# Tile 0's attention reordered, and the halves of the first weight blocks given to other engines and slots

## The reference

```python
scores = scale * q @ k.T                    # 2 batches, 8 heads, 768 rows, head size 64
keep = (key < n_global) | ((0 <= row - key) & (row - key < n_local))   # 8 and 96
a = softmax(where(keep, scores - slope[h] * dist, -1e9))
x = (a @ v)                                 # laid out as 1536 x 512
h = x @ w_in                                # 512 -> 1024
s = h * softmax(h)
y = (s - mean(s)) / sqrt(var(s) + 1e-6) * g_ln @ w_out      # 1024 -> 512
yn = y / sqrt(mean(y * y) + 1e-6) * rms_g
out = (silu(yn @ w_gate) * (yn @ w_val)) @ w_down           # 512 -> 1536 -> 512
```

## Time and profile before

| what | value |
|---|---|
| median of 3 runs | 596.89 us (596.87 to 596.99) |
| profiled execution, its own time | 597.28 us |
| its span | 595.5 us |
| PE busy | 575.6 us (97%) |
| DVE, ACT, POOL busy | 303.3, 258.4, 83.5 us |
| mean granted clock of PE | 0.977 |

### The profile page before, as it was taken

How to read it: one execution, slowest core, us unless ns; L and a number is a source line. 1 busy time by engine, 2 the same in 40 slices (tenths; PEclk the granted TensorE clock), 3 DMA queues, 4 the chain that set the end, 5 groups by cost and what they waited for, 6 DMA issues and landing times.

```text
span 595.5 us, 10886 instructions
## 1 busy us (share of the span) xinstructions
PE 575.6 (97%) x3787; PEld 520.8 (87%) x3787; DVE 303.3 (51%) x778; ACT 258.4 (43%) x598; POOL 83.5 (14%) x223
## 2 busy tenths in 40 slices
PE   6967999999999999999999999999999999999997
PEld 6956888888888888878899999999999999999996
DVE  5757878777877898767455213222222222221211
ACT  3655656665665677646454212222221222222112
POOL 4440220222112205213010010001001000100000
PEclk9796799999999999999999999999999999999999
DMA  8664454432443343232532100020020000000000
GB/s 215 188 187 139 128 172 124 137 109 77 124 125 108 91 126 99 81 133 89 181 108 85 58 16 1 1 72 1 1 70 0 0 0 35 0 0 36 2 0 36
DMA packets 21614, 46.97 MB, mean 79 GB/s; under 512 B 2764, under 2 KB 2776, under 8 KB 21576
## 3 DMA queue, kind: packets, MB, share of 16 engines
q1 hardware_dynamic: 21264, 46.47, 25.9%
q10 hardware_dynamic: 312, 0.01, 0.0%
HBM read 40.18 MB, written 6.29 MB: 78 GB/s over the span
## 4 chain that ended last, share of the span: by engine, by line
PE 81%; DVE 9%; POOL 4%; issue 3%; ACT 2%; DMA 1%; ACTq 0%; DVEq 0%; SPq 0%
PE hidden L412 9%; PE hidden L413 9%; PE hidden L414 8%; PE mixed L1248 5%; PE turned L412 3%; PE turned L413 3%; PE mixed L412 3%; PE mixed L413 3%; PE scores_b L412 3%; PE scores_a L413 3%; PE scores_b L413 3%; PE scores_a L412 3%; PE turned L414 3%; PE scores_a L414 3%; PE scores_b L414 3%
## 5 line engine op out<-in xcount | busy, mean ns | idle before, releaser
L733 ACT ACTIVATE act_hi<-act_sb 128x256 fp32r<-128x256 f32 x72 | 30.2, 419 | 108.7 <-DVE act_sb L1106 108.7
L1106 DVE TENSOR_TENSOR act_sb<-mixed,silu 128x256 f32<-128x256 f32 x36 | 15.3, 425 | 93.3 <-PE mixed L414 93.1
L1106 DVE TENSOR_TENSOR act_sb<-turned,silu 128x256 f32<-128x256 f32 x36 | 15.3, 424 | 89.3 <-PE turned L414 86.8
L1248 PEld LDWEIGHTS mixed<-v_in,probs_t 116*128 116x128 f32 x384 | 53.4, 203 | 7.8 <-ACT probs_t L684 4.2
L684 ACT ACTIVATE probs_t<-turned 116x512 f32<-116x512 f32 x48 | 28.7, 598 | 67.6 <-PE turned L1233 67.5
L412 PE MATMUL hidden<-down_hi,act_hi 128*128 128x512 f32 x144 | 56.9, 395 | 0.1
L413 PE MATMUL hidden<-down_lo,act_hi 128*128 128x512 f32 x144 | 56.9, 395 | 0.0
L414 PE MATMUL hidden<-down_hi,act_lo 128*128 128x512 f32 x144 | 56.7, 393 | 0.0
L1248 PE MATMUL mixed<-v_in,probs_t 116*128 116x64 f32 x384 | 51.7, 281 | 3.4 <-ACT probs_t L684 3.4
L1111 DVE TENSOR_TENSOR act_lo<-act_sb,act_hi 128x256 fp32r<-128x256 f32 x72 | 30.6, 425 | 35.0 <-ACT act_hi L733 35.0
L674 ACT ACTIVATE probs<-logits,neg_max 128x232 f32<-128x232 f32 x96 | 45.8, 483 | 3.8 <-DVE neg_max L997 3.8
(11 more groups left out here) (147 smaller groups left out, 1567.5 us busy)
## 6 DMA issues: line engine op xcount, KB each, us to landing
qk_raw<-qk_pairs SPq DMA_DIRECT2D x96, 180.0 KB, 3.2
v_in<-v_windows SPq DMA_DIRECT2D x12, 448.0 KB
staging<-w_gate SPq DMA_DIRECT2D x3, 1024.0 KB, 7.3
staging<-w_val SPq DMA_DIRECT2D x3, 1024.0 KB, 5.8
y_spill<-y_out SPq DMA_DIRECT2D x12, 256.0 KB, 4.2
staging<-w_down SPq DMA_DIRECT2D x3, 1024.0 KB, 5.7
y_in<-y_spill SPq DMA_DIRECT2D x6, 512.0 KB, 4.0
out<-o_sb SPq DMA_DIRECT2D x12, 256.0 KB, 2.1
```

What stands on the lines that cost most here:

```text
L733: nc.scalar.activation(act_hi[:, slot], act_sb[:, slot], ACT.Copy).then_inc(act_rounded, 1)
L1106: nc.vector.tensor_tensor(act_sb[:, slot], val_ps[slot][:, 0:WIDE], silu[:, slot], ALU.mult).then_inc(act_ready, 1)
L1248: ins = pe.matmul(mixed[:, head * d:(head + 1) * d], probs_t[:, p % 2, h, half], v_in[:, even, half, head * d:(head + 1) * d], start=(half ...
```

## The change

- SP's queue begins with the DMA of n_local, which was ACT's second.
- `find_general` is the first thing that DVE computes after the bounds; ACT reads the flag before tile 0's first exp, not after it.
- In `one_tile(-1)` PE issues, for each pair, the scores of the next pair, 3 fillers, the transposes, 1 filler and the mix. Before it was transposes, scores, 3 fillers, mix, 3 fillers. In front of that, 6 fillers stand for 3.
- SP loads block 1 at the start of `one_tile(-1)` and not at its end.
- Blocks 0 and 1 are each split half by DVE and half by POOL. POOL does block 0's second half between the fourth and the fifth of the 8 biases, and block 1's second half behind them. DVE did both halves of block 0 before, POOL both of block 1.
- The four roundings of w_out, and so their splits on DVE, stand one pair later.
- `take_logits` of tile 1 waits for the two biases of its own pair and not for all eight.

```diff
@@ one_tile on PE
-                        turn_pair(n, p)
                         score_pair(n + 1, (p + 1) % pairs)
                         keep_busy(FILL)
+                        turn_pair(n, p)
+                        keep_busy(1)
                         mix_pair(a, 1 - even, p)
-                        keep_busy(FILL)
                         continue
@@ the start of PE
             score_pair(0, 0)
-            keep_busy(FILL)
+            keep_busy(2 * FILL)
@@ slots of roundings and splits
         round_1 = {(-1, 1): [(0, 0)], (-1, 2): [(0, 1)], (0, 0): [(1, 0), (1, 1)],
-                   (0, 2): [(2, 0)], (0, 3): [(2, 1)], (1, 0): [(3, 0)], (1, 1): [(3, 1)],
+                   (0, 3): [(2, 0)], (1, 0): [(2, 1)], (1, 1): [(3, 0)], (1, 2): [(3, 1)],
...
-        del split_1[0, 1]
+        del split_1[-1, 3]
+        split_1[0, 1] = [(1, 0)]
@@ POOL
+            def split_half(c):
+
+                hi, lo, raw, _ = half_block(c, 1)
+                pool.wait_ge(w_rounded, 2 * c + 2)
+                pool.tensor_tensor(lo, raw, hi.bitcast(F32), ALU.subtract).then_inc(w_in_split[c], 1)
...
-            for half in range(2):
-                hi, lo, raw, _ = half_block(1, half)
-                pool.wait_ge(w_rounded, 2 * 1 + half + 1)
-                pool.tensor_tensor(lo, raw, hi.bitcast(F32), ALU.subtract).then_inc(w_in1_split, 1)
+                if h == heads // 2 - 1:
+                    split_half(0)
+            split_half(1)
@@ SP
+            sp.dma_start(bounds_i[:, 1, :], n_local.bitcast(I32).partition_broadcast(P)).then_inc(bounds_in, 16)
...
+                if known(t) and t < 0:
+                    load_block(sp, 1)
                 for p in range(pairs):
...
-                if known(t) and t < 0:
-                    load_block(sp, 1)
@@ ACT
-            for i, n in enumerate((n_global, n_local)):
-                act.dma_start(bounds_i[:, i, :], n.bitcast(I32).partition_broadcast(P)).then_inc(bounds_in, 16)
+            act.dma_start(bounds_i[:, 0, :], n_global.bitcast(I32).partition_broadcast(P)).then_inc(bounds_in, 16)
...
-            exp_pair(0, 0, 0)
             act.wait_ge(general_known, 1)
             general = act.value_load(general_i[0:1, 0:1], min_val=0, max_val=1)
             with act.If(general != 0):
                 general_attention()
+            exp_pair(0, 0, 0)
@@ DVE
-                if known(n) and n == pairs:
-                    dve.wait_ge(bias_others, heads)
+                if known(n) and pairs <= n < 2 * pairs:
+                    dve.wait_ge(bias_others, 2 * (p + 1))
...
+            find_general()
             start_distance(0)
             split_qk(0, 0)
             finish_distance(0)
             set_bias()
             take_logits(0, 0, 0)
-            find_general()
             split_qk(1, 1)
```

More of the change, by code:

```diff
@@ L215, in fused_kernel @@
         w_split = sem("w_split")
-        w_in1_split = sem("w_in1_split")
+        w_in_split = [sem("w_in0_split"), sem("w_in1_split")]
         qk_loaded = [sem(f"qk_loaded_{p}") for p in range(pairs)]
@@ L337, in wait_split @@
         def wait_split(engine, c):
-            if c == 1:
-                engine.wait_ge(w_in1_split, 2)
+            if c < N1:
+                engine.wait_ge(w_in_split[c], 2)
             else:
-                engine.wait_ge(w_split, 2 if c == 0 else 2 * c)
+                engine.wait_ge(w_split, 2 * (c - N1 + 1))
         def load_block(sp, c):
@@ L387, in split_block @@
             if gain is None:
-                nc.vector.tensor_tensor(lo, raw, hi, ALU.subtract).then_inc(w_split, 1)
+                nc.vector.tensor_tensor(lo, raw, hi, ALU.subtract
+                                        ).then_inc(w_in_split[c] if c < N1 else w_split, 1)
                 return
@@ L846, in _, with find_general @@
                                            in1=bounds_f[:, :, 0], op0=ALU.mult, op1=ALU.add).then_inc(setup, 1)
+            def find_general():
+                dve.wait_ge(setup, 3)
+                nc.vector.tensor_scalar(general_f[:], bounds[:, 0:1], float(GLOBAL), None, ALU.is_gt).then_inc(setup, 1)
+                dve.wait_ge(setup, 4)
+                nc.vector.scalar_tensor_tensor(out=general_f[:], in0=bounds[:, 1:2], scalar=float(PREV + 1),
+                                               in1=general_f[:], op0=ALU.is_gt, op1=ALU.max).then_inc(setup, 1)
+                dve.wait_ge(setup, 5)
+                nc.vector.scalar_tensor_tensor(out=general_i[:], in0=bounds[:, 1:2], scalar=1.0,
+                                               in1=general_f[:], op0=ALU.is_lt, op1=ALU.max).then_inc(general_known, 1)
             DIST_STEPS = 7
-            DISTANCE = (3, 12)
             def start_distance(v):
-                at = DISTANCE[v]
+                at = 5 + DIST_STEPS * v
                 dve.wait_ge(iota_done, 7)
@@ L883, in set_bias @@
                                             ).then_inc(bias_first, 1)
[L885 to L893, removed]
             def general_attention():
```

## The result

The changed kernel took 603.33 us (median of 6, 599.68 to 605.16). Beside it the kernel before took 596.83 (median of 6); the ratio is 1.0107, with a 95% interval of 1.0069 to 1.0146. That is slower, as forecast, but by 6.4 us and not by 2.3, and outside the range. Timed beside the later variants the kernel before had medians of 595.3 to 596.2, lower than the three runs shown ahead of the prediction. So medians of different comparisons can't be subtracted to better than 1 or 2 us, and the ratios are the safe figures: 0.001 of ratio is 0.6 us.

The account below looks back on a forecast made before the run. PE was taken to bound the kernel from 80.57 us on, its milestones and clock deciding before; -0.6 + 1.8 - 3.4 - 2.5 + 0.5 + 3.3 + 3.2 = +2.3 gave 599.2 us, range 594.3 to 601.3.

Parts of the forecast that it names:

- The start: Before tile 0's attention: pair 1's scores come first at 12.9, clock low from 14.6 to 21.4 as before.
- Tile 0's attention: Up to tile 0's turn_x: it comes at 30.6 us, -0.6 us, with bounds of -1.8 and 0.
- The meeting: Tile 0: DVE's subtractions of pair 5 meet POOL's split of block 0's second half and end 0.9 us after it.
- Block 1 and the clock: Tile 0's turn_x to block 1's products: clock falls near 31.6, rises near 41.9; block 1 at 42.0; +1.8 and -3.4 us.
- the -3.4: Behind block 1's first product: dense work that ran at half clock until 48.7 now runs at full clock, -3.4 us.
- rival (d): Near 38.4: POOL's copy into bias_even blocks DVE's split of pair 7, block 1 1.4 us later; +3.7, 600.6 us; chance 0.10.
- (c): Rival, tile 0: the clock's low stretch isn't swapped; +4.0 in all, 600.9 us; chance 0.18.
- The out block: Up to tile 1's turn_x: block 2's rounding leaves ACT's path (1.2) and its split DVE's (1.3), -2.5 us.
- Given back at tile 2: Tile 2's turn_x: waits for SP's issues behind load_block(5), held by the last w_out split; +3.3 us, bounds +1.3 and +3.4.
- +0.5: Behind tile 1's turn_x: PE's dense stretch starts earlier at low clock, whose low part is 1.1 us longer; +0.5 us.
- The clock at tile 2: Behind tile 2's turn_x: the clock falls once more after PE's idle time; +3.2 us, bounds 0 and +6.8.
- Block 1's own term: Block 1's first product: at 42.0, 1.2 us later than 40.84; against the -0.6 of tile 0's attention, +1.8 us.

Follow-up runs that it names:

- the old slots: The changed kernel with the four roundings and splits of w_out back one pair earlier, as before the change: 599.82 us, ratio 1.0075 to the kernel before.
- the copy late: The changed kernel with POOL's copy into bias_even held until both halves of block 1 are split: 600.40 us, ratio 1.0078 to the kernel before.
- block 5 late: The changed kernel with SP's load_block(5) behind finish_x of tile 2, not at the end of tile 1: 596.29 us, ratio 1.0027 to the kernel before.
- the control: The kernel before with load_block(5) behind tile 2's finish_x on SP, tiles 2 and 3 written out on SP's program: 596.19 us, ratio 1.0009.
- the slots alone: The kernel before with only the four roundings and splits of w_out one pair later: 601.17 us, ratio 1.0097.

## Why the prediction was right and wrong

**The start.** The order was right: pair 1's scores came at 12.82 (12.9 predicted), before the transposes. Two readings were not. The 3.16 us before 13.38 can't have been mostly the read of the flag. In the trace of the kernel before, the flag was written only at 12.06, so at most 1.3 us of them were:

```profile
...
11.81 0.25 DVE L892 SCALAR_TENSOR_TENSOR general_i<-bounds,general_f 128x1 int32<-128x1 f32 x1
...
```

And the clock's first low stretch wasn't the old one (14.6 to 21.4), but lay from 13.1 to 16.5.

**Tile 0's attention.** -0.6 predicted, -1.26 measured at turn_x (29.98). The meeting came as described: POOL's half ran 25.34 to 27.71 and DVE's k_lo, ready at 25.98, took 2.23 us and ended 0.50 after it. But the size of the gain was luck. POOL began 0.7 us sooner than forecast after a start in which the clock was low for 3.4 us and not 6.8. The runs with the old slots and with the copy late have the same programs up to here, and their clock was low for 6.8 us; POOL began at 26.55 and 26.85, and turn_x stood at 31.17 and 31.47, no earlier than the 31.24 before. The profile of the changed kernel, then of the one with the old slots; the mean granted clock from 12 to 24 us is 0.86 and 0.72:

```profile
...
12.00:24.00 12.00, 9.99 (x69) 9.32 (x70) 9.08 (x29) 7.79 (x20) 6.78 (x8) 0.86 1.05 292
...
```

```profile
...
12.00:24.00 12.00, 10.68 (x64) 10.06 (x64) 8.00 (x27) 6.56 (x17) 6.75 (x8) 0.72 1.05 293
...
31.17 0.96 PE L1268 MATMUL turned_x<-ident,x 128*128 128x128 f32 x4 [2.04 <-SPq L496]
...
```

With the clock that the forecast assumed, this term was about 0.

**Block 1 and the clock.** This is the step that failed. The fall near 31.6 came (30.2), in idle time without fillers. But the -3.4 for the dense work behind block 1 did not: the clock rose at 37.0 already, PE then ran at full rate into the wait for block 1, stood 2.69 us there, and the clock fell a second time, for 6.8 us as in the old kernel. Two low stretches, not one moved. The wait was long for two reasons. With the clock up at 37.0 PE was at block 1 at 39.8, not at 41.5. And rival (d) came true: DVE's subtraction of pair 7 took 2.10 us beside POOL's copy. I had given the copy 1.4 us and a clock that isn't swapped another rival, (c), with a chance each, as if they were separate. In the profile of the run with the copy held back the wait is 1.3 us shorter and the second fall is gone, so the copy's 1.3 us can decide on the clock's 3.4. They don't in every execution: in the profile with block 5 late the copy met DVE too, but the clock was low until 41.7, PE waited 0.36 us, and there was no second fall. With the old slots the copy and the clock together took 4.7 us by the medians, as much as the sum of the two.

The Trainium skill (SBUF — State Buffer, "Who interferes with whom") calls this meeting an exclusive lock, and not shared bandwidth. The runs agree: the subtraction (0.64 in free time) ended 0.50 us behind POOL's copy, and that of pair 5 ended 0.50 behind POOL's split of block 0. Why that is less than its own 0.64 they don't show. With the copy held back it took 0.79, and 0.64 in the profile with the old slots as well, where POOL was idle beside it. Beside POOL's short instructions (232 elements a row, 0.8 to 0.9 us each) no profile has it above 0.83: it is the long rows that cost.

**The out block.** -2.5 predicted at tile 1's turn_x, 1.8 measured by undoing the slots. Mis-sized a little: the 1.3 of DVE's split came, but of ACT's 1.2 only 0.5. In the old trace DVE had waited no longer than that for ACT's rounding of pair 8:

```profile
...
52.40 0.64 DVE L972 TENSOR_TENSOR k_lo<-qk_raw,qk_hi 128x464 fp32r<-128x464 f32 x1 [0.47 <-ACT qk_hi L664]
...
```

With the rounding out of the way DVE went on right behind pair 8's logits, which wait for PE's scores.

**Given back at tile 2.** +3.3 predicted, and +0.5 for the low clock ahead of it, 3.8 together for this stage; 3.3 measured (25.27 against 21.95). The +0.5 (1.3 us and not 1.1 longer by its own figures: 53.9 to 62.4 against 58.62 to 65.8) was wrong in sign: of the stage, 6.2 us lay at low clock (58.14 to 64.3) where it was 7.2 before, so the wait itself gave back about 3.8. SP issued block 5 at 79.60 and had passed x on by 83.41, 3.8 us later; x alone, ready at 80.79, would have allowed 81.0. The run with block 5 late shows the cause, and so does the control, in which the same edit gained nothing where SP wasn't in the way.

**The clock at tile 2.** +3.2 predicted for turn_x of tile 2 to that of tile 3, 2.7 measured (23.12 against 20.42 in the old trace). All three profiled kernels with an idle time of 3.9 us here had a low stretch behind it; none of the ten others, with 0 to 1.5, had one.

**The rest.** Of the 6.5 us, 5.5 are there at tile 3's turn_x. The last 1.0 is lost between 318 and 344 us, in the first block of the second feed-forward part, where PE waits for act_lo once for 0.8 us. Other variants lose 0.3 to 1.5 us at the same place. I did not test why; it stays open.

So four terms held within 0.7 us, the first of them by luck: tile 0's attention, the out block, tile 2's wait with the +0.5 taken to it, and its clock. Block 1's own term was 1.1 too small (+1.8, and +2.9 from 40.84 and 31.24 to 42.48 and 29.98), and the -3.4 was a gain of which, beside that of the out block, 0.3 came. These two and the 1.0 of the rest are 5.2 us; the smaller misses take 1.0 back, which leaves the 4.2 between +2.3 and +6.5.

**The median.** Two of the six runs (599.68 and 599.96) lie within 1 us of the forecast, the other four at 602.9 to 605.2. The variant with block 5 late falls into two groups in the same way. Only one run of each kernel was profiled, so that the fast ones are those without a second fall in tile 0 is likely but not shown.

## What to carry to other kernels

When a piece of work is moved later, look up who waits for it in an in-order DMA queue, and count everything that stands between that wait and the next thing that the critical engine needs; here one issue, moved by a few places, was worth 4 to 5 us. An idle time on PE has two prices, its length and the low clock that may follow, and the second can be the larger: whether 1.3 us of a wait go or stay may decide on 3.4 more, so the two belong into one case and not into two independent ones. POOL's instructions over long rows (1024 and 1856 elements) held DVE's two-input subtractions here until they had ended, so place such an instruction where DVE has none. And when two profiles are compared, look first whether the clock had the same pattern ahead of the place in question: here tile 0's turn_x stood at 29.1 us without a low stretch in the start, at 30.0 with one of 3.4 us and at 31.2 to 31.5 with one of 6.8, for one and the same program up to there.

## What was unexpected of the hardware

The clock's edges lie at other times in each execution. Three profiled kernels share the start of the kernel before (it, the slots alone, and the control); PE resumed at 13.3 to 13.4 us in all three, and the first fall stood at 14.6, 11.3 and 13.1. Of the nine with the start of the changed one, five had it at 12.7 to 14.3 and four had no low stretch there at all. Each low stretch lasted about 3.4, 6.8, 10.2 or 13.7 us. That goes with the spread of the totals: one kernel's runs lay 2 to 7 us apart (599.7 to 605.2 for the changed one, 594.2 to 598.6 for the kernel before in one comparison). Of the twelve runs with block 5 late, eight had a mean granted clock of 0.980 to 0.983 and took 595.2 to 597.8 us; four had 0.974 to 0.977 and took 598.7 to 600.3. Three runs of a kernel were too few to fix its median to 1 us.
